# Second weights of a gated scan and ELU feed-forward kernel: four matrices of a pair stored column beside column

## What is computed

```
f = lower_bound + (1 - lower_bound) * sigmoid(f_logit)
h[t] = f[t] * h[t-1] + (1 - f[t]) * x[t]            # x: 2 x 6080 x 256
y = h.reshape(12160, 256)
u = y @ w_in                                         # w_in: 256 x 2048
g = where(u > 0, u, exp(min(u, 0)) - 1)
out = g @ w_out                                      # w_out: 2048 x 256
```

## Time and profile before

| | |
|---|---|
| Runs | 990.57 us (median of 3; 990.54 to 991.19) |
| The profiled execution | 990.41 us |
| its span, first to last instruction | 988.6 us |
| TensorE matmuls | 4362, of these 18 bfloat16 ones as warm-up |
| Weight loads | 4362, one for each matmul |

### The profile page before, as it was taken

The page is one execution under the profiler, slowest core; times in us unless marked ns, Lnnn a source line. Parts: engine busy times, 40 slices in busy tenths (PEclk is TensorE's granted clock), DMA queues, the critical chain, the costliest instruction groups (busy, mean ns, idle before and its releaser), DMA issues.

```text
span 988.6 us, 15352 instructions
## 1 busy us (share of the span) xinstructions
PE 982.2 (99%) x4362; PEld 817.1 (83%) x4362; DVE 728.0 (74%) x915; ACT 793.0 (80%) x1425; POOL 631.9 (64%) x474
## 2 busy tenths in 40 slices
PE   8999999999999999999999999999999999999998
PEld 5888888888888888888888888888888888888997
DVE  6896876886786697688679668758867957875544
ACT  7988878878887887888788788788788788778775
POOL 2686887567657557656755855765675675576454
PEclk9999999999999999999999999999999999999999
DMA  7102002101201100210210120021021012000001
GB/s 277 64 23 74 33 1 76 54 1 53 74 0 42 53 32 0 74 53 0 64 64 0 42 64 21 21 55 52 0 71 56 0 46 70 0 0 13 33 1 38
DMA packets 23211, 41.88 MB, mean 42 GB/s; under 512 B 2704, under 2 KB 4240, under 8 KB 23184
## 3 DMA queue, kind: packets, MB, share of 16 engines
q1 hardware_dynamic: 22752, 41.04, 12.8%
q10 hardware_dynamic: 432, 0.53, 0.2%
HBM read 29.10 MB, written 12.45 MB: 42 GB/s over the span
## 4 chain that ended last, share of the span: by engine, by line
PE 99%; DMA 1%; DVE 0%; ACTq 0%; ACT 0%; issue 0%
PE acc L866 17%; PE acc L864 17%; PE acc L865 17%; PE h L838 14%; PE h L840 14%; PE h L836 14%; PE h L961 1%; PE h L959 1%; PE h L960 1%; DMA x<-value 1%; PE h L940 0%; DVE x L603 0%; PE h L931 0%; PE acc L961 0%; PE acc L959 0%; PE acc L940 0%
## 5 line engine op out<-in xcount | busy, mean ns | idle before, releaser
L317 POOL TENSOR_TENSOR g_lo<-e,g_hi 128x512 fp32r<-128x512 f32 (+1 forms) x384 | 519.4, 1362 | 351.0 <-ACT g_hi L458 349.5
L444 ACT ACTIVATE e<-h 128x512 f32<-128x512 f32 (+1 forms) x380 | 226.0, 595 | 151.4 <-PE h L840 129.3
L694 DVE SCALAR_TENSOR_TENSOR e<-e,h 128x512 f32<-128x512 f32 (+1 forms) x380 | 256.8, 676 | 70.3 <-ACT e L450 70.0
L866 PE MATMUL acc<-g_hi,w_out_lo 128*128 128x512 f32 (+1 forms) x768 | 297.3, 387 | 0.0
L864 PE MATMUL acc<-g_hi,w_out_hi 128*128 128x512 f32 (+1 forms) x768 | 297.3, 387 | 0.0
L865 PE MATMUL acc<-g_lo,w_out_hi 128*128 128x512 f32 (+1 forms) x768 | 297.2, 387 | 0.0
L450 ACT ACTIVATE e<-e 128x512 f32<-128x512 f32 (+1 forms) x384 | 241.5, 629 | 8.4
L458 ACT CAST g_hi<-e 128x512 fp32r<-128x512 f32 (+1 forms) x384 | 232.4, 605 | 16.9 <-DVE e L694 16.9
L838 PE MATMUL h<-a_lo,w_in_hi 128*128 128x512 f32 (+1 forms) x616 | 238.4, 387 | 0.0
L836 PE MATMUL h<-a_hi,w_in_hi 128*128 128x512 f32 (+1 forms) x616 | 238.2, 387 | 0.0
L840 PE MATMUL h<-a_hi,w_in_lo 128*128 128x512 f32 (+1 forms) x616 | 238.2, 387 | 0.0
(11 more groups left out here) (72 smaller groups left out, 564.6 us busy)
## 6 DMA issues: line engine op xcount, KB each, us to landing
out<-out_sb SPq DMA_DIRECT2D x44, 256.0 KB, 2.0
gate<-forget_logit SPq DMA_DIRECT2D x43, 256.0 KB, 2.6
x<-value SPq DMA_DIRECT2D x43, 256.0 KB, 2.7
w_in_raw<-w_in SPq DMA_DIRECT2D x8, 256.0 KB, 6.2
w_out_raw<-w_out SPq DMA_DIRECT2D x8, 256.0 KB, 7.1
x<-value SPq DMA_DIRECT2D x4, 224.0 KB, 2.5
gate<-forget_logit SPq DMA_DIRECT2D x4, 224.0 KB, 2.5
out<-out_sb SPq DMA_DIRECT2D x4, 224.0 KB, 1.9
```

The lines of the kernel that those rows point to most:

```text
L317: nc.gpsimd.tensor_tensor(g_lo[:, t % RING, 0:w], e[:, t % TILES, 0:w], g_hi[:, t % RING, 0:w].bitcast(F32), ALU.subtract).then_inc(g_lo_r ...
L444: nc.scalar.activation(e[:, i, 0:w], bank_of(j, t)[:, 0:w], ACT.Relu, scale=-1.0).then_inc(r_ready, 1)
L694: nc.vector.scalar_tensor_tensor(e[:, t % TILES, 0:w], e[:, t % TILES, 0:w], -1.0, bank_of(j, t)[:, 0:w], ALU.add, ALU.max).then_inc(g_rea ...
L866: done = nc.tensor.matmul(bank, lo, g_hi[:, t % RING, 0:w], start=False, stop=closes)
```

## The change

The four matrices of a pair are interleaved: for each of the 128 columns of a matrix, a partition holds the four values of (u = 0, half 0), (u = 0, half 1), (u = 1, half 0), (u = 1, half 1). The arrays become `[P, PAIRS, P, 2, HALVES]`, the host lays `w_out` out in the same way, and a weight matrix is read as 128 floats with a step of four floats, 16 bytes. Transfers, rounding and remainder still go over whole pairs.

```diff
-        w_out_raw = nc.alloc_sbuf_tensor_at("w_out_raw", [P, PAIRS, 2, D], F32, offset=w_out_at)
-        w_out_lo = nc.alloc_sbuf_tensor_at("w_out_lo", [P, PAIRS, 2, D], F32R, offset=w_out_at)
+        w_out_raw = nc.alloc_sbuf_tensor_at("w_out_raw", [P, PAIRS, P, 2, HALVES], F32, offset=w_out_at)
+        w_out_lo = nc.alloc_sbuf_tensor_at("w_out_lo", [P, PAIRS, P, 2, HALVES], F32R, offset=w_out_at)
...
-        w_out_hi = sb("w_out_hi", [P, PAIRS, 2, D], F32R)
+        w_out_hi = sb("w_out_hi", [P, PAIRS, P, 2, HALVES], F32R)
...
-                cols = slice(half * P, (half + 1) * P)
-                hi, lo = w_out_hi[:, q, u, cols], w_out_lo[:, q, u, cols]
+                hi, lo = w_out_hi[:, q, :, u, half], w_out_lo[:, q, :, u, half]
...
         "w_out": np.ascontiguousarray(
-            moe_w_out.reshape(PAIRS, 2, P, D).transpose(0, 2, 1, 3)),
+
+            moe_w_out.reshape(PAIRS, 2, P, HALVES, P).transpose(0, 2, 4, 1, 3)),
```

## The result

The changed kernel took 1019.88 us (median of 4 runs, 1019.30 to 1020.13) against 990.56 for the kernel before on the same chip: a ratio of 1.0294 (95% interval 1.0276 to 1.0312), 29.3 us slower. The profiled execution took 1019.69 us, with a span of 1017.9, so the two spans show the whole difference (1017.9 - 988.6 = 29.3).

What follows compares the result with a forecast made beforehand. TensorE was taken as the bound: number of matmuls times start-to-start distance. Parts (1) to (3) cost 0, part (4) gains 20 us: 990.41 - 20 = 970.4, said 970. Range: gain (963 to 977), no change, and more meetings up to 1030.

Steps and rivals of the forecast that it cites:

- more meetings: Rival, chance 0.20: at second products each new 16-byte piece opened holds up the matmul 3.4 ns; excess doubles, 31 us lost.
- What bounds the kernel, the count and the distances: TensorE's matmuls times start-to-start distance: 2112 second products of 512 columns at 226.7 ns, 192 of 448 at 202.7.
- Parts (1) to (3): Host layout, load of `w_out`, rounding by ScalarE and remainder by VectorE: 0 each; bound about 2 us lost.
- part (4): The 2304 second-product weight loads read 128 floats with a step of four: 15.6 to 25 us gained, 20 taken.
- the excess comes from meetings: Matmul time above its columns (10.7 ns over the warm-up's 216) arises where weight load and data stream meet in memory.
- shorter stays mean less excess: Second products: a strided load stays a quarter as long on each 16-byte piece, so at most half the excess stays.
- The read of 108 ns: After a float32 weight load the next can begin after about 108 ns, half of the 226.7 ns it has.
- The three sizes: Matmuls of 448 columns in the last block recorded at 362, 365 or 369 ns, read as steps of 3 to 4 ns.
- The bare 213.3 ns: Time of 512 columns alone at 2.4 GHz, leaving an excess of 13.3 ns; at 448 columns 186.7, excess 16.0.
- the load becomes the bound: Rival, chance 0.12: each strided second-product load takes 0.296 us and sets the distance; 164 us lost, about 1155.
- no change: Rival, chance 0.25: the excess belongs to float32 streams, a strided load up to 226.7 ns stays hidden; 990.6, up to 993.
- wrong altogether: Sign against the whole prediction: first products changing with the second ones, or VectorE and ScalarE as releasers of TensorE.

Runs made afterwards that it cites:

- alone_contig: Kernel before, contiguous layout, with the middle matmul of each second product cut to 32 columns (its correction left out for the others): 923.60 us.
- alone_step16: Changed kernel, step of 16 bytes, with the middle matmul of each second product cut to 32 columns (its correction left out for the others): 1020.59 us.

## Why the prediction was wrong

The forecast was 970 us, a gain of 20; measured is a loss of 29.3. The stated range held 1019.88 only because it held a rival, "more meetings".

- **What bounds the kernel, the count and the distances** held: no new wait, and 29.2 of the 29.3 us in distances of TensorE, 22 of them in the 2304 second products.
- **Parts (1) to (3) at nothing** held: the rounding (L483) takes 612 ns and the remainder (L665) 752 (medians; 613 and 756 before), and TensorE's waits are no longer.
- **The step that failed is part (4)**, the gain of 15.6 to 25 us, in two places. First, both gains supposed that a strided load reads a weight in the same 0.84 ns, so that it would stay on a piece for less time. It reads at half that speed: 214 ns alone instead of 108 (115 at two weights for 16 bytes). Second, the step from "the excess comes from meetings" to "shorter stays mean less excess" does not follow. The step of 8 bytes tests it with a load that is almost as fast as the contiguous one (115 ns against 108): by the count of weights for each piece the stays are halved, and the distance at 512 columns is 233 instead of 226.7 ns. That the excess hangs on more than the columns was right (empty bytes alone move it); that it consists of meetings stays an inference, and the rows gave no sign, gain or loss, for its price. The distance of 226.7 ns, 10.7 over the 216 of the warm-up, was already the smallest at 512 columns of the five places tried.
- **The numbers behind part (4)**, held against the traces. The read of 108 ns held: in the trace of before, the load of L931 at 8.234 us is followed by the next at 8.342, and two more such pairs are 108 ns apart too, each load recorded with 186 to 191 ns; alone_contig has 108 again (median of 704), and that is half (48%) of the 226.7 ns. The three sizes held as recorded in that one trace: of its 321 matmuls from 920 to 985 us, 64 have 362 ns, 192 have 365 and 65 have 369, and all 3167 from 182 to 900 us have 389. As a rule of steps they did not hold: with 32 empty bytes the matmuls of 182 to 900 us have 393, 394, 396 and 397 ns, a quarter each, and 352 of the 360 of 448 columns have 369, beside loads of 187 to 188 ns. That the steps are the load's stay on four weights was an estimate from 108 / 128, and no run shows it. The bare 213.3 ns was an estimate as well: the warm-up's distances are 426 to 427 ns from 1.73 to 3.86 us and 215 to 216 from 4.18 us on, which is 1.20 and 2.37 columns in a nanosecond, and 213.3 is half of the first. No row shows a clock in GHz, and the stretches of 1.30 to 4.00 us and 4.18 to 6.20 us both have a granted clock of 1.00. Measured is the excess of 10.7 ns over 216; the 13.3 and the 16.0 rest on the estimate.
- **The rival "the load becomes the bound"**, given 0.12, is what happened, at 448 columns alone and at 512 together with the place. Its price was mis-sized: it took a chain of 0.296 us for each load, read plus whole recorded length; measured are 234 ns at both widths, so that 164 us become 22 (15.9 + 5.9). The doubling to 216 ns, in the "no change" rival, was right to 2 ns; what went wrong there is the cover. After a strided load, whose read lets the next begin after 214 ns, its matmul goes only after some 0.24 us, more than the 226.7 that were to hide it.
- **"More meetings", 1021 us**, came within 1.1 us by accident. It had 240 ns at 512 columns (measured 234.2) and 202.7 + 16.0 = 219 at 448 (measured 233.7), by a hold-up of the stream, and these misses nearly cancel with the 7.4 us of the first products, which it left alone; with 256 columns fewer the strided distances did not shrink (470 ns for two, against 469). At the step of 8 bytes (233.2 ns with a read of 115) a hold-up of the stream is the reading that is left, an inference too.
- **No term at all** stood for the first products: 7.4 us. Their steady 226.7 ns is a state that a strided load beside or just ahead of them disturbs (230.9 and 232.5 ns), and a shortened matmul too (median 231 ns, contiguous, 256 columns). What sets it stays open. The prediction had called a change there "wrong altogether".

## What to carry to other kernels

Keep a float32 weight row contiguous: one weight for each 16 bytes doubled the read of a 128-column load here (214 ns against 108), and even two for each 16 bytes cost 16 us (1006.79 against 990.44) without the load being a bound. Compare a load's read plus the delay behind it with the matmul beside it, not the read alone (here 243 ns and not 214, against 226.7); the sum of two distances around a shortened matmul measures that. In a kernel with TensorE busy throughout, try a few offsets between the weights and the data early: here 32 and 96 empty bytes cost 28 us of 990.

## What the runs showed that I had not expected

Empty bytes between buffers change every matmul's distance (226.7 to 233.4 ns at 512 columns, 200.0 to 206.7 at 448), although loads are recorded the same; 64 bytes is better at 448 columns than before (200.0 against 203.0 ns for second products) and worse at 512. A step of 32 bytes is slower than one of 16 for the load alone (228 against 214 ns), so the count of 16-byte pieces, 128 in both, is not the whole price. And a matmul's start is recorded before its weights are there (in alone_step16 the load runs from 529.97 to 530.28 us and its matmul is recorded from 529.99): with a late load the wait is in the length of its record (0.51 and 0.60 us above) and in the distance to the next start, not in the distance from the start before. So a single distance is not always what its own matmul costs.
